# Attention in front of a mixture of experts: q, k and v arrive turned and in tile order, and the head loop is written out

## What is computed

```python
scores = (q @ k.T) / sqrt(64)
thresh = max(scores, axis=-1) - tau
scores = where(scores >= thresh, scores, -1e9)
attn   = exp(scores - max(scores))
attn   = attn / (sum(attn) + 1e-9)
out    = attn @ v
```

## Time and profile before

| | |
|---|---|
| median of 3 runs | 1323.1 us (1320.86 to 1324.55) |
| profiled execution | 1323.5 us, of which its span is 1321.7 us |
| TensorE busy | 1258.8 us, 95% of the span |
| VectorE busy | 643.6 us, 49% |
| ScalarE busy | 539.7 us, 41% |
| GpSimd busy | 522.0 us, 39% |
| attention, to its last GpSimd low part | about 375 us of the span |

### The profile page before, as it was taken

How to read it: one execution, slowest core, us unless ns; L and a number is a source line. 1 busy time by engine, 2 the same in 40 slices (tenths; PEclk the granted TensorE clock), 3 DMA queues, 4 the chain that set the end, 5 groups by cost and what they waited for, 6 DMA issues and landing times.

```text
span 1321.7 us, 22228 instructions
## 1 busy us (share of the span) xinstructions
PE 1258.8 (95%) x7838; PEld 1155.7 (87%) x7838; DVE 643.6 (49%) x1279; ACT 539.7 (41%) x962; POOL 522.0 (39%) x377
## 2 busy tenths in 40 slices
PE   4999999999985999999999999998999999999998
PEld 3999999999864889989999999997999999899997
DVE  5789889889745511212111121216454535444433
ACT  2688888778753233333323333333211112111211
POOL 0677787777830253443435344354421101000000
PEclk9999999999987999999999999999999999999999
DMA  5555555555340052333424243344321102000000
GB/s 134 120 136 133 133 124 141 132 132 132 93 140 24 30 178 94 130 117 109 142 95 143 73 150 104 120 151 128 96 68 52 33 0 73 16 0 24 16 1 24
DMA packets 112492, 123.65 MB, mean 94 GB/s; under 512 B 56752, under 2 KB 75440, under 8 KB 112432
## 3 DMA queue, kind: packets, MB, share of 16 engines
q1 hardware_dynamic: 98560, 87.70, 23.8%
q0 software_dynamic: 6080, 19.93, 4.8%
q10 hardware_dynamic: 7792, 15.21, 3.1%
HBM read 81.90 MB, written 19.92 MB: 77 GB/s over the span
## 4 chain that ended last, share of the span: by engine, by line
PE 79%; DVE 5%; POOL 4%; ACT 4%; issue 4%; DMA 3%; SPq 0%; POOLq 0%; ACTq 0%; DVEq 0%
PE h_ps L709 31%; PE y_ps L728 10%; PE y_ps L727 10%; PE y_ps L726 10%; PE o_acc L567 5%; POOL probs_lo L1303 3%; PE ring L528 2%; PE ring L529 2%; PE ring L542 2%; PE ring L541 2%; PE t_ps L687 2%; DMA q_lo<-k_parts 1%; ACT probs_hi L804 1%; DMA k_parts<-k_ones 1%; POOL region_a L1309 1%
## 5 line engine op out<-in xcount | busy, mean ns | idle before, releaser
L709 PE MATMUL h_ps<-x_hi,region_a 128*128 128x384 f32 (+1 forms) x1408 | 342.0, 315 | 5.3 <-DVE x_lo L1200 4.3
L1303 POOL TENSOR_TENSOR probs_lo<-probs,probs_hi 128x576 fp32r<-128x576 f32 x160 | 226.4, 1428 | 77.7 <-ACT probs_hi L804 77.7
L709 PEld LDWEIGHTS h_ps<-x_hi,region_a 128*128 128x128 f32 x1408 | 244.9, 188 | 12.0 <-DVE x_lo L1200 5.1
L709 PE MATMUL h_ps<-x_lo,region_a 128*128 128x384 f32 (+1 forms) x704 | 220.3, 313 | 0.0
L1210 DVE SCALAR_TENSOR_TENSOR h_lo<-h_ps,h_hi 128x256 fp32r<-128x256 f32 (+1 forms) x128 | 62.8, 491 | 310.5 <-ACT h_hi L898 287.3
L901 ACT ACTIVATE h_hi<-act_out 128x384 fp32r<-128x384 f32 (+1 forms) x112 | 53.9, 481 | 312.2 <-DVE act_out L1221 309.4
L726 PE MATMUL y_ps<-region_b,h_hi 128*128 128x512 f32 x448 | 175.8, 392 | 1.4 <-DVE h_lo L1227 1.4
L727 PE MATMUL y_ps<-region_b,h_hi 128*128 128x512 f32 x448 | 176.6, 394 | 0.0
L728 PE MATMUL y_ps<-region_b,h_lo 128*128 128x512 f32 x448 | 176.5, 394 | 0.0
L1218 DVE TENSOR_SCALAR act_neg<-h_ps,alpha_sb 128x384 f32<-128x384 f32 (+1 forms) x112 | 62.7, 560 | 186.7 <-PE h_ps L709 185.8
L1289 POOL TENSOR_TENSOR region_b<-stage,region_b 128x1024 fp32r<-128x1024 f32 x40 | 95.8, 2399 | 144.0 <-ACT region_b L785 143.9
(11 more groups left out here) (200 smaller groups left out, 2429.8 us busy)
## 6 DMA issues: line engine op xcount, KB each, us to landing
stage<-in_moe_w SPq DMA_DIRECT2D x56, 512.0 KB
expert_rows<-rows_out ACTq DMA_DIRECT2D x8, 768.0 KB, 3.9
k_ones<-q_hi SPq DMA_DIRECT2D x32, 160.0 KB, 2.7
q_lo<-k_parts SPq DMA_DIRECT2D x32, 160.0 KB, 2.6
q_hi<-q_hi SPq DMA_DIRECT2D x32, 160.0 KB, 2.4
k_parts<-k_ones SPq DMA_DIRECT2D x32, 160.0 KB, 2.7
qk_nat<-in_q SPq DMA_DIRECT2D x32, 128.0 KB, 2.7
qk_nat<-in_k SPq DMA_DIRECT2D x32, 128.0 KB, 2.9
```

Source lines behind the costliest of these rows:

```text
L709: mm = pe.matmul(h_ps[:, c % 2, 0:width], wt, x[kind][:, cc, :], start=(n == 0), stop=(n == 3 * C - 1))
L1303: pool.tensor_tensor(probs_lo[:, m % 4, :], probs[:, m % 4, :], probs_hi[:, m % 4, :].bitcast(F32), ALU.subtract).then_inc(lo_done, 1)
```

## The change

The host lays q and k out turned, 64 rows of q over 64 rows of k by 640 columns in the kernel's tile order, with the tail's 64 columns twice, in one tensor `qk`; v comes in tile order too. The kernel loads them as they are: one load per head for q and k (into `qk_raw`), one load per pair for v. TensorE's transposes and their use of a ring place are gone. ScalarE's copy and VectorE's subtraction read `qk_raw` in SBUF. The loads of v of the first four heads move up to the start, right behind those of q and k, and the threshold's load moves behind the first pair. Five of the memsets move from VectorE to GpSimd, and the one for the tail rows of `qk_nat` is gone. The hardware loop over iterations 1 to 6 is written out.

```diff
-        qk_nat = sb("qk_nat", [P, 2, 2, NT, 2 * D])
+        qk_raw = sb("qk_raw", [P, 2, 2, SP])
...
         def slots(eng, slot):
-            for n in range(FIRST, SL):
+            for n in range(FIRST, LAST):
                 slot(n // SL, n % SL)
-            with eng.Fori(1, TILES // SL - 1) as i:
-                for c in range(SL):
-                    slot(i, c)
-            for n in range(TILES - SL, LAST):
-                slot(n // SL, n % SL)
...
+        def parts_split(eng, heads):
+            wait(eng, qk_lo_done, heads)
...
-        numbers = {"s": {}, "st": {}, "qk": {}, "om": {}}
+        numbers = {"s": {}, "st": {}, "om": {}}
...
-            sp.dma_start(threshold[:, :], tau.partition_broadcast(P)).then_inc(tau_in, 16)
...
             def load_pair(i, c):
-                wait(sp, qk_turned, h0 - U + 2)
-                for g in range(2):
-                    for n, src in enumerate((qh, kh)):
-                        sp.dma_start(qk_nat[:, pair, g, 0:FULL, n * D:n * D + D],
-                                     src[bass.ds(h0 + g, 1), 0:FULL * P, :].rearrange("h (p t) d -> p (h t) d", p=P)).then_inc(qk_in[pair], 16)
-                sp.wait_ge(padded, 1)
-                for n, src, at in ((0, qh, 0), (1, kh, 0), (1, kh, TAIL)):
-                    sp.dma_start(qk_nat[at:at + TAIL, pair, :, FULL, n * D:n * D + D],
-                                 src[bass.ds(h0, 2), FULL * P:S, :].rearrange("h p d -> p h d")).then_inc(qk_in[pair], 16)
+                parts_split(sp, h0 - U + 2)
+                for lane in range(2):
+                    sp.dma_start(qk_raw[:, pair, lane, :], qkh[h0 + lane]).then_inc(qk_in[2 * pair + lane], 16)
...
             def load_v_pair(i, c):
-                (3 loads)
+                sp.dma_start(v_nat[:, pair, :, :, :].rearrange("p g t d -> p g (t d)"),
+                             vh[h0:h0 + 2].rearrange("h p n -> p h n")).then_inc(v_in[pair], 16)
...
             load_pair(0, 0)
+            sp.dma_start(threshold[:, :], tau.partition_broadcast(P)).then_inc(tau_in, 16)
             load_pair(0, 2)
-            sp.wait_ge(consts_v, 4)
+            load_v_pair(0, 0)
+            load_v_pair(0, 2)
...
-                    wait(sp, freed, past("qk", i, g))
+                    parts_split(sp, head(i, g) + 1)
                     sp.dma_start(q_lo[0:D, s, :].bitcast(F32), k_parts[0:D, s, :].bitcast(F32)).then_inc(parts_in[g % 2], 16)
...
-                if isinstance(i, int) and tile(i, c) == -6:
-                    load_v_pair(0, 0)
-                    load_v_pair(0, 2)
...
         # TensorE
-                g = turned_in(i, c)
-                if g is not None and has(i, g, NH, U):
-                    place_free(pe, "qk", i, g)
-                    wait(pe, qk_in[pair], (head(i, g - g % U) // U + 1) * 16 * 7)
-                    flat = ring[:, place("qk", i, g)].rearrange("p a n -> p (a n)")
-                    for t in range(NT):
-                        mm = pe.transpose(flat[:, t * P:t * P + P], qk_nat[:, pair, lane, t, :], ident[:, :])
-                    mm.then_inc(qk_turned, 1)
...
         # ScalarE
-                    wait(act, qk_turned, head(i, g) + 1)
+                    wait(act, qk_in[g % U], (head(i, g) // U + 1) * 16)
                     wait(act, st_ready, tile(i, (g - U) * NT + NT))
-                    act.activation(q_hi2[:, g % U, :], ring[:, place("qk", i, g)].rearrange("p a n -> p (a n)")[:, 0:SP],
-                                   ACT.Copy).then_inc(qk_hi_done, 1)
+                    act.activation(q_hi2[:, g % U, :], qk_raw[:, g % U // 2, g % 2, :], ACT.Copy).then_inc(qk_hi_done, 1)
...
         # VectorE
-            dve.memset(qk_nat[:, :, :, FULL, :], 0.0).then_inc(padded, 1)
-            dve.memset(neg_max[:, :, :, :].bitcast(F32), 0.0)
+            dve.memset(v_lo[0:TAIL, :, FULL, D:D + 1].bitcast(F32), 1.0)
+            dve.memset(v_lo[TAIL:P, :, FULL, D:D + 1].bitcast(F32), 0.0)
             dve.memset(q_lo[D:D + 4, :, :].bitcast(F32), 0.0)
-            dve.memset(max_cols[:, :, 0:D + 2].bitcast(F32), 0.0)
-            dve.memset(o_t[:, :, :], 0.0)
-            dve.memset(k_ones[D:D + 4, :, :].bitcast(F32), 1.0)
+            dve.memset(k_ones[D:D + 4, :, :].bitcast(F32), 1.0).then_inc(max_row_consts, 1)
...
-                    dve.tensor_tensor(k_parts[:, s, :], ring[:, place("qk", i, g)].rearrange("p a n -> p (a n)")[:, 0:SP],
-                                      q_hi2[:, s, :].bitcast(F32), ALU.subtract).then_inc(freed, 1)
+                    dve.tensor_tensor(k_parts[:, s, :], qk_raw[:, s // 2, s % 2, :], q_hi2[:, s, :].bitcast(F32),
+                                      ALU.subtract).then_inc(qk_lo_done, 1)
...
         # GpSimd
+            pool.memset(v_lo[:, :, 0:FULL, D:D + 1].bitcast(F32), 0.0)
+            pool.memset(v_hi[:, :, :, D:D + 1].bitcast(F32), 1.0)
+            pool.memset(neg_max[:, :, :, :].bitcast(F32), 0.0)
+            pool.memset(max_cols[:, :, 0:D + 2].bitcast(F32), 0.0)
+            pool.memset(o_t[:, :, :], 0.0).then_inc(consts_v, 1)
...
         # host
+    order = [p * full + t for t in range(full) for p in range(P)] + [t for _ in range(2) for t in range(rest, S)]
+    turned = lambda a: a[:, :, order, :].transpose(0, 1, 3, 2)
+    laid["qk"] = _np.concatenate([turned(inputs["q"]), turned(inputs["k"])], axis=2)
+    laid["v"] = inputs["v"][:, :, order, :].reshape(B, H, full + 1, P, D).transpose(0, 1, 3, 2, 4).reshape(B, H, P, (full + 1) * D)
```

More of the change, by code:

```diff
@@ L14, with build @@
 I32 = mybir.dt.int32
-def build(nc, q, k, v, tau, w_gate, w_noise, noise, w1, w2, w_in, w_out, alpha, out):
-    B, H, S, D = q.shape
+def build(nc, qk, v, tau, w_gate, w_noise, noise, w1, w2, w_in, w_out, alpha, out):
+    B, H = qk.shape[:2]
+    S, D = out.shape[0] // B, qk.shape[2] // 2
     NH = B * H
@@ L46, in build @@
     RAW = NCH * CH
-    qh = q.rearrange("b h s d -> (b h) s d")
-    kh = k.rearrange("b h s d -> (b h) s d")
-    vh = v.rearrange("b h s d -> (b h) s d")
+    qkh = qk.rearrange("b h r s -> (b h) r s")
+    vh = v.rearrange("b h p n -> (b h) p n")
     x_dram = nc.dram_tensor("x_rows", (B * S, H * D), F32, kind="Internal").ap()
@@ L102, in build @@
         o_acc = ps("o_acc", [P, 2, 512])
-        consts = sem("consts"); consts_v = sem("consts_v"); padded = sem("padded")
+        consts = sem("consts"); consts_v = sem("consts_v"); max_row_consts = sem("max_row_consts")
         first_w_in = sem("first_w_in"); first_w_hi = sem("first_w_hi"); first_w_lo = sem("first_w_lo"); tau_in = sem("tau_in")
-        qk_in = [sem(f"qk_in{i}") for i in range(2)]
+        qk_in = [sem(f"qk_in{i}") for i in range(U)]
         v_in = [sem(f"v_in{i}") for i in range(2)]
-        qk_turned = sem("qk_turned"); qk_hi_done = sem("qk_hi_done")
+        qk_hi_done = sem("qk_hi_done"); qk_lo_done = sem("qk_lo_done")
         parts_in = [sem(f"parts_in{i}") for i in range(2)]
@@ L292, in has @@
         def has(i, c, total, per):
[L294 removed]
+            return 0 <= i * per + c < total
         def wait(eng, s, count):
@@ L340, in max_rows_in @@
             return c // NT + 1 if c % NT == 3 else None
-        numbers = {"s": {}, "st": {}, "qk": {}, "om": {}}
+        numbers = {"s": {}, "st": {}, "om": {}}
         for n in range(FIRST, LAST):
-            g = turned_in(n // SL, n % SL)
             f = max_rows_in(n // SL, n % SL)
-            for kind, m, total in (("s", n + AHEAD, TILES), ("st", n, TILES), ("qk", -1 if g is None else n // SL * U + g, NH),
+            for kind, m, total in (("s", n + AHEAD, TILES), ("st", n, TILES),
                                    ("om", -1 if f is None else n // SL * U + f, NH + 2)):
@@ L349, in build @@
                     numbers[kind][m] = sum(len(v) for v in numbers.values())
-        USES = 2 * SL + 2 * U
         def use(kind, i, c):
[L354 to L357, removed]
+            return numbers[kind][i * (SL if kind in ("s", "st") else U) + c]
         def past(kind, i, c):
-            return 0 if isinstance(i, int) and i * (SL if kind in ("s", "st") else U) + c < 0 else use(kind, i, c) + 1
+            return 0 if i * (SL if kind in ("s", "st") else U) + c < 0 else use(kind, i, c) + 1
         def place(kind, i, c):
-            per = SL if kind in ("s", "st") else U
-            return (numbers[kind][i * per + c] if isinstance(i, int) else numbers[kind][per + c]) % 3
+            return use(kind, i, c) % 3
         def place_free(eng, kind, i, c):
@@ L512, in _ @@
             pe.wait_ge(consts, 2)
-            pe.wait_ge(consts_v, 4)
+            pe.wait_ge(consts_v, 3)
+            pe.wait_ge(max_row_consts, 1)
             def slot(i, c):
@@ L788, in slot @@
                 j = c % NT
-                g = turned_in(i, c)
+                g = split_in(i, c)
                 f = max_rows_in(i, c)
@@ L816, in slot @@
                     pair, lane = h % U // 2, h % 2
-                    wait(act, v_in[pair], (head(i, h - h % U) // U + 1) * 16 * 3)
```

(11 more changed lines are left out.)

25 lines of the change are left out of this document (8 added, 17 removed).

## The result

The changed kernel takes 1326.75 us in the median (1323.72 to 1328.07, 9 runs), the kernel before 1323.26 us in the same session (1320.86 to 1326.16, 9 runs). The ratio is 1.0021, 95% interval 1.0012 to 1.0030: slower by 0.2%, where 1313.5 us were forecast, outside the range of 1301 to 1320. The profiled execution has a span of 1325.1 us, 3.4 us more than before.

What follows compares the result with a forecast made beforehand. TensorE was taken to set the pace, with GpSimd the bound for a moment in split heads. 6.2 (start) + 8.3 (transposes) - 4.9 (hold) = 9.6 us off 1323.5 gave 1313.9, median 1313.5; range 1301 to 1320.

Steps and rivals of the forecast that it cites:

- the hold behind a split: In 14 heads with a weight split, k_parts and GpSimd's region_a meet; GpSimd loses 0.35 us each, 4.9 us (bounds 0, 9.8).
- the transposes: Five per head leave TensorE; 0.55 us gained in each of 15 heads, none behind splits: 8.3 us (bounds 8.3, 16.0).
- the loop: Writing out the head loop gives nothing, since its branch costs nothing on this path, and extra instruction fetching costs 0.
- VectorE's 2.5 us a group: VectorE held about 1.25 us in each split head; 37.99 + 2.5 = 40.5 of 42.46 us, so VectorE carries it.
- The heads without a split: Heads where GpSimd splits no expert weights: 0.55 us gained in each of 15, q_hi starts 9.9 to 10.1 us apart.
- the one ring place less: Turned q and k no longer take one of three PSUM ring places; TensorE hardly waits for one, so worth 0.
- the sign that the prediction itself named for being wrong: TensorE's waits in the steady part going to a ring place, with VectorE late, would show the prediction wrong.
- The split heads themselves: Behind weight splits, TensorE without transposes only arrives earlier and waits longer for GpSimd: 0 gained.
- The start: Fewer VectorE memsets, no transposes, earlier third-head copies: TensorE restarts 6.2 us earlier (bounds 3 and 7.5).
- ScalarE's source: ScalarE's q_hi copy, 0.71 us from PSUM, reads SBUF instead; with 8 us of slack a group, taken as 0.
- D: Rival: k_parts meets a running GpSimd low part in every head; 19.5 us slower, 1342.6 us; chance 0.06.
- C: Rival: k_parts waits through region_a and GpSimd's next operation, 2.66 us; 1323 us, no change; chance 0.10.

Runs made afterwards that it cites:

- Experiment 1: Changed kernel, with VectorE's k_parts subtraction replaced by a reduction over the same 640 columns with one SBUF input (low parts left out): 1316.2 us, ratio 0.9952.
- experiment 4: Kernel before, transposes kept, with VectorE's k_parts subtraction reading unturned q and k in SBUF instead of the turned ones in PSUM: 1329.5 us, ratio 1.0052.
- experiment 5: Kernel before, with only the head loop written out: 1321.2 us, ratio 0.9992.
- experiment 14: Changed kernel, with v's first loads moved back to slot -6: 1324.3 us, ratio 1.0015 to the kernel before.
- experiments 6: Changed kernel, with VectorE's k_parts subtraction one slot later, in slot 2: 1339.0 us, ratio 1.0123 to the kernel before.
- 7: Changed kernel, with k_parts in slot 2 and the weight splits in slots 8 and 13: 1343.6 us, ratio 1.0157 to the kernel before.
- 9: Changed kernel, weight splits in slots 8 and 13, k_parts behind the first maximum of slot 2: 1327.7 us, ratio 1.0036 to the kernel before.
- 11: Changed kernel, weight splits in slots 8 and 13, ScalarE's q_hi copy in slot 0 instead of 1: 1337.6 us, ratio 1.0111 to the kernel before.
- the late splits: Changed kernel, with the weight splits of ScalarE and GpSimd in slots 8 and 13 instead of 5 and 10: 1312.5 us, ratio 0.9915 to the kernel before.
- experiments 14 to 17: Besides experiment 14, three kernels with the late splits and first loads reordered: alone 1311.3 us; k_parts on GpSimd 1313.6; that plus q_hi in slot 0, 1309.1.

## Why the prediction was wrong

Two steps failed: the hold behind a split was priced too low, and the transposes were booked as a gain in heads where they gave little or nothing. A third term, the loop, was put at 0 and gave 2.3 us. From the fifth q_hi copy to the last, 3.4 us of gain were forecast (8.3 - 4.9) and 4.9 of loss measured.

**The hold behind a split.** The mechanism was right: the place (region_a and k_parts), the 14 heads, VectorE's 1.25 us, and that GpSimd is held in turn. The size of the term was not. I took 0.35 us a head for GpSimd, the middle between 0 and one whole subtraction. Measured are +0.69 and +0.64 us in the two heads of a group. Experiment 1 puts 0.57 and 0.64 of it on the hold, 8.6 us in 14 heads instead of 4.9; experiment 4 gives 0.53 to 0.60 for it alone. That is what GpSimd itself loses, 0.58 us in the low part or 0.64 in region_a. VectorE's 2.5 us a group, which I let it carry because its sum of work, 40.5 us, fitted into 42.46, aren't free either: in the heads where k_parts is held, the maximum that frees TensorE's place and the threshold that GpSimd's low part needs come late. But the heads where VectorE isn't held are as long, so its lateness isn't needed for the loss. The page "SBUF — State Buffer" of the Trainium skill, section "Who interferes with whom", says that the one that starts first holds the other for its whole length; the trace shows both directions (1.98 us for VectorE at 85.37, 1.93 us for GpSimd at 96.72), and the 8.6 us are nearer to the upper bound, 9.8, than to the half that I took.

**The heads without a split** were to gain 0.55 us each, 8.3 us. Forecast were intervals of 9.9 to 10.1 us. They are 0.2 us shorter than before (10.57 and 10.48 to 10.33 and 10.29), and experiment 5 gives that to the loop: written out, with the transposes kept, such heads take 10.31 and, undisturbed, 10.32. I had read the freed 0.55 us as wholly TensorE's, and the one ring place less as worth 0. What the runs show in its place is that TensorE waits for a ring place instead, the sign that the prediction itself named for being wrong. They stay at 10.30 with one input, so no hold is in it. The chain goes over exponential, threshold, k_parts and maximum; moving q_hi takes 0.14 off, moving k_parts makes it worse. That the rest is the latency of that chain over ScalarE and VectorE is argued, not shown.

**The loop** was costed at nothing, from one interval of 10.57 us held against heads of both kinds. Against the other heads without a split it was long: 10.33 us is what the one written-out interval from slot 16 to 1 took. From the fifth q_hi copy to the last, experiment 5 is 2.3 us shorter than the kernel before. Experiment 1, without transposes and with the new loads, is 1.4 us shorter than experiment 5, all but 0.1 of it in the interval from slot 1 to 6; the hold costs 8.6. Together that is the 4.9 us of loss.

**The split heads themselves:** I took no gain there because GpSimd is the bound. With the hold away (experiment 1) they take 10.77, as before (10.64 and 10.77; 10.76 in experiment 5): right.

**The start** was forecast at 6.2 us and gave 4.0. The memsets and transposes gave their 4.1 (q_hi at 6.61, forecast 6.6). The first copy behind 1920 KB lost 2.1 us, where I allowed 0 to 1: I counted the queue empty near 8 us, but v's last load landed at 12.07, and the copy issued at 8.34 landed at 12.87. The third head's scores came at 29.59, forecast 27.4. That the 2.1 us are what is missing isn't shown: experiment 14 takes them away in the first copy and gains only 0.4 at the fifth q_hi.

**Costed at nothing:** ScalarE's source was right (0.73 instead of 0.71 us). In the heads without a split GpSimd is held too, as the prediction allowed: a low part takes 1.66 us instead of 1.43, and since experiment 1 doesn't shorten these heads, it costs nothing there. The lighter issuing of SP was not tried alone.

**Not forecast:** the stretch behind the last q_hi took 0.8 us more, and what lies behind the attention 1.8 us more. Over all kernels here that last part varies between 942.9 and 946.9 us with one code, so I don't hang a cause on it; whether the change has a part in it stays open.

**The rivals.** D named a low part met in every head as the way to a slower kernel. The changed kernel doesn't do that, but experiments 6, 7, 9 and 11 do, at 1327.7 to 1343.6 us. C didn't occur: k_parts never waited through two GpSimd operations, and took 1.98 us where it was held.

Summed by what was measured in the profiled execution: -4.0 for the start, +4.9 for 27 heads (+8.6 in the 14 with a split, -3.7 in the 13 others), +0.8 and +1.8 behind, which is +3.4 before rounding.

## What to carry to other kernels

Before a VectorE operation is given a second SBUF input, lay its place over GpSimd's timeline, instruction by instruction; the sum of both engines' work doesn't show what a meeting costs, and in a periodic kernel a meeting happens in every period. Moving one of the two can be free (the late splits took the ratio from 1.0021 to 0.9915), but only if the new place is laid over the timeline too: k_parts one slot later gave 1.0123. Putting both on one engine avoided the question (0.9893, and 0.9869 with the q_hi copy moved), even at twice the time for the operation. When work is taken off the engine that sets the pace, look for the second longest chain within one step of the pipeline, not for the engine with the second most work. When several things change at once, try those costed at nothing alone too, and look into the trace even where the total doesn't move: here the loop had the gain that would have been put down to the transposes.

## What the runs showed of the hardware

VectorE and GpSimd held each other wherever a VectorE subtraction with two SBUF inputs met a GpSimd subtraction. The one that is held ends a fixed time behind the other's end, a little less than it takes alone: k_parts 0.68 to 0.69 us behind (0.81 alone; 1.98 in the changed kernel), region_a 1.14 (1.29 alone; 1.93 to 1.96 in all), a low part 1.26 to 1.30 (1.43 alone; 1.66 to 2.0 in all). A reduction with one SBUF input over the same 640 columns was never held (0.81 us in all heads), nor did it hold GpSimd (low parts at 1.42 us). An operation whose two inputs are a PSUM place and an SBUF tile was not held either, in 32 heads of the kernel before (0.812 to 0.825 us). With VectorE's start 0.02 us behind GpSimd's or later, k_parts was held; with it 0.02 us ahead, region_a; where the two starts in the trace lay within about 0.01 us, both occurred.

A DMA from SBUF to SBUF of 160 KB, the first of the start, took 2.37 to 2.41 us from issue to landing in the four kernels without v's loads in the queue ahead of it (experiments 14 to 17), and 2.68 to 4.58 us in the eleven kernels with them.

The intervals in the kernel before were 10.54 to 10.58 us from slot 16 to 1 across the hardware loop's branch, and 10.31 to 10.35 us in the same place with the loop written out.
